# Attention, Fourier mixing and two feed-forward layers on one core: unrounded products gathered into three groups in the attention's loop

## The reference

```python
# batch 2, heads 8, sequence 768, head size 64
q_bits = (np.einsum('bhsd,dk->bhsk', q, proj) > 0)      # 6 bits each
k_bits = (np.einsum('bhsd,dk->bhsk', k, proj) > 0)
mask = q_bucket[:, :, :, None] == k_bucket[:, :, None, :]
scores = np.where(mask, scale * np.matmul(q, k.transpose(0, 1, 3, 2)), -1e9)
scores = scores - np.max(scores, axis=-1, keepdims=True)
attn = np.exp(scores)
attn = attn / (np.sum(attn, axis=-1, keepdims=True) + 1e-09)
out = np.matmul(attn, v)
# then: x = Fourier transform over tokens and features (real part), layer norm, 512 -> 2048 -> 512 feed-forward
# then: 512 -> 1024, gelu, gate mixed over the 768 tokens, 512 -> 512, residual
```

## Time and profile before

| what | value |
|---|---|
| median of 3 runs | 731.67 us (729.86 to 733.08) |
| profiled execution | 731.51 us, its span 729.7 us |
| TensorE, weight loads | 98%, 81% busy |
| VectorE, ScalarE, GpSimd | 66%, 52%, 48% busy |

### The profile page before, as it was taken

The page is one execution under the profiler, slowest core; times in us unless marked ns, Lnnn a source line. Parts: engine busy times, 40 slices in busy tenths (PEclk is TensorE's granted clock), DMA queues, the critical chain, the costliest instruction groups (busy, mean ns, idle before and its releaser), DMA issues.

```text
span 729.7 us, 11758 instructions
## 1 busy us (share of the span) xinstructions
PE 715.2 (98%) x3905; PEld 589.8 (81%) x3905; DVE 479.7 (66%) x701; ACT 382.3 (52%) x708; POOL 348.4 (48%) x341
## 2 busy tenths in 40 slices
PE   8999999999999999999999999999999998999998
PEld 8857666766676899988888888999998887888886
DVE  6877878778875799976555677444434774347533
ACT  4877887788785535554445445444541553025300
POOL 4178878887887910134533162536533353005500
PEclk9999999999999999999999999999999999999999
DMA  4332323332334140031211212721003000010001
GB/s 97 67 77 65 80 56 76 68 74 58 73 81 124 47 151 1 18 100 58 58 59 58 58 57 88 252 65 57 30 1 145 0 1 1 29 58 1 0 15 73
DMA packets 71076, 45.20 MB, mean 62 GB/s; under 512 B 44996, under 2 KB 61560, under 8 KB 70520
## 3 DMA queue, kind: packets, MB, share of 16 engines
q1 hardware_dynamic: 70456, 41.19, 20.7%
q0 software_dynamic: 576, 3.43, 1.4%
HBM read 35.42 MB, written 3.15 MB: 53 GB/s over the span
## 4 chain that ended last, share of the span: by engine, by line
PE 86%; DVE 8%; POOL 2%; ACT 2%; issue 1%; DMA 1%; SPq 0%; POOLq 0%; ACTq 0%; DVEq 0%
PE PS L811 81%; DVE un L2011 2%; DVE mneg L1773 1%; PE PS L835 1%; PE PS L1098 1%; PE PS L1315 1%; PE PS L1269 1%; DMA ops<-mrow 1%; PE PS L950 1%; PE PS L1260 1%; DVE st L1999 0%; DVE W1L L2044 0%; DVE ops L1744 0%; DVE ops L1765 0%; DVE ops L1738 0%
## 5 line engine op out<-in xcount | busy, mean ns | idle before, releaser
L811 PE MATMUL PS<-ops 98*128 98x384 f32 (+1 forms) x576 | 134.7, 359 | 3.4 <-DMA ops<-mrow 1.1
L811 PEld LDWEIGHTS PS<-ops 98*128 98x128 f32 (+1 forms) x576 | 95.2, 189 | 44.2 <-ACT E L1383 19.6
L1773 DVE TENSOR_REDUCE mneg<-PS 128x1 f32<-128x768 f32 x96 | 91.5, 956 | 36.8 <-PE PS L811 36.1
L1383 ACT ACTIVATE E<-PS 128x384 f32<-128x384 f32 x192 | 83.4, 486 | 44.6 <-PE PS L811 43.8
L661 POOL TENSOR_TENSOR esum<-esum,E 128x768 f32<-128x768 f32 x56 | 102.6, 1832 | 2.8 <-ACT E L1383 0.3
L646 POOL TENSOR_TENSOR W2L<-W2R,W2H 128x1024 fp32r<-128x1024 f32 x16 | 38.8, 2428 | 111.8 <-ACT W2H L1367 111.8
L2060 DVE SCALAR_TENSOR_TENSOR hL<-pre,hH 128x384 fp32r<-128x384 f32 x42 | 43.8, 1043 | 51.1 <-ACT hH L1628 51.1
L811 PE MATMUL PS<-BH,W1H 128*128 128x384 f32 x228 | 76.8, 337 | 0.4 <-DVE hL L2060 0.2
L811 PE MATMUL PS<-BH,W1L 128*128 128x384 f32 x228 | 76.8, 337 | 0.0
L811 PE MATMUL PS<-BL,W1H 128*128 128x384 f32 x228 | 76.1, 334 | 0.0
L811 PE MATMUL PS<-W2H,hH 128*128 128x512 f32 x192 | 75.5, 393 | 0.0
(11 more groups left out here) (211 smaller groups left out, 1595.4 us busy)
## 6 DMA issues: line engine op xcount, KB each, us to landing
W1R<-in_moe_w_ch_dram SPq DMA_DIRECT2D x32, 256.0 KB, 3.2
W2R<-in_moe_w_ch_dram SPq DMA_DIRECT2D x32, 256.0 KB, 3.0
ops<-ops SPq DMA_DIRECT2D x30, 192.0 KB, 3.0
qk<-in_k_dram SPq DMA_DIRECT2D x32, 96.0 KB, 2.5
qk<-in_q_dram SPq DMA_DIRECT2D x32, 96.0 KB, 2.6
vn<-in_v_dram SPq DMA_DIRECT2D x32, 96.0 KB, 2.5
out_dram<-X SPq DMA_DIRECT2D x12, 256.0 KB, 2.0
WsgR<-in_moe_w_sg_dram SPq DMA_DIRECT2D x1, 2304.0 KB, 8.0
```

Source lines behind the costliest of these rows:

```text
L811: return pe.matmul(dst, lhs, rhs, start=start, stop=stop, **kw)
L1383: act.activation(A["E"][:, e_slot(t, 0, kt), half(a)], PS[:, ST_BANK + a, 0:HALF], ACT.Exp, scale=EXP_SCALE).then_inc(exp_done, 1)
L1773: dve.tensor_reduce(A["mneg"][:, s, j:j + 1], PS[:, bank:bank + 2, 0:HALF], AX.XY, ALU.max, negate=True).then_inc(max_done, 1)
```

## The change

Two of the functions are changed, TensorE's and ScalarE's `one_time`, in the order of their steps alone. In TensorE's round the last max pair of head `t+1` goes ahead of the transposes, the denominators of head `t-1` go from behind the first max pair of head `t+2` to right behind the first part of the values, and the turn-back goes from the round's end to ahead of the second part of the values. In ScalarE's round the copy of the keys goes behind the third exponentials (tile 2), and the copy of the sums ahead of the fourth (tile 3) instead of behind them.

```diff
                 if t.has(0):
                     scores(t, 0, 2)
+                if t.has(1):
+                    scores_for_max(t, 1, 5)
                 if t.has(3):
                     transposes(t, 3)
-                if t.has(1):
-                    scores_for_max(t, 1, 5)
                 if t.has(0):
                     values(t, 0, 0)
+                if t.has(-1) and not late(t, -1):
+                    denominators(t, -1)
+                if t.has(0):
                     scores(t, 0, 3)
                 if t.has(2):
                     scores_for_max(t, 2, 0)
-                if t.has(-1) and not late(t, -1):
-                    denominators(t, -1)
                 if t.has(0):
                     scores(t, 0, 4)
...
                 if t.has(2):
                     scores_for_max(t, 2, 1)
+                if t.has(-1) and not late(t, -1):
+                    turn_back(t, -1)
                 if t.has(0):
                     values(t, 0, 1)
                     scores(t, 0, 5)
                 if t.has(2):
                     scores_for_max(t, 2, 2)
-                if t.has(-1) and not late(t, -1):
-                    turn_back(t, -1)
...
                 if t.has(2):
                     mask_rows(t, 2, 1)
-                if t.has(3):
-                    upper_keys(t, 3)
                 if t.has(0):
                     exponentials(t, 2)
                 if t.has(3):
+                    upper_keys(t, 3)
                     upper_queries(t, 3)
                 if t.has(1):
                     split_upper(t, 1)
+                if t.has(-1) and not late(t, -1):
+                    raw_sums(t, -1)
                 if t.has(0):
                     exponentials(t, 3)
-                if t.has(-1) and not late(t, -1):
-                    raw_sums(t, -1)
```

## The result

The changed kernel takes 737.73 us (median of 4, 737.32 to 739.26) against 730.76 for the kernel before on the same chip: ratio 1.0095, 95% interval 1.0078 to 1.0111. It is slower by 7.0 us; 739.2 was forecast, 7.5 above the median shown.

The account below looks back on a forecast made before the run. TensorE alone was taken to bound the attention loop. Terms -0.34 - 0.21 + 0.60 + 0.31 + 0.25 = +0.61 us a round, +7.3 in 12 rounds, +0.3 in the tail: 739.2 us forecast, range 735.0 to 743.0.

Parts of the forecast that it names:

- Bound: Attention loop, heads 1 to 12: each nanosecond TensorE saves or waits is a nanosecond of the kernel, twelve times over.
- Group price, -0.34: Denominators merged behind the values' first part on TensorE: one 64-wide group fewer saves its fixed price, 0.34 us a round.
- Rows' wait, -0.21: Scores behind the turn-back: with the sums' copy earlier, the wait for the rows' DMA goes, saving 0.21 us a round.
- Q+5.7: Next head's first scores: the maxima's rows arrive 5.7 us after scores 3 start; TensorE comes at 6.0, so no wait.
- Sixth maximum, +0.60: Sixth max pair on TensorE: waits for VectorE's reduction of the fifth, 0.50 plus 0.10 unhidden load, +0.60 us a round.
- Scores 4, +0.31: Scores 4 on TensorE: wait for exponentials 3 to free their bank, +0.31 us a round, bounds 0.14 and 0.40.
- Q+0.81: ScalarE: exponentials 3 start 0.81 us after scores 3 start, behind the sums' copy that now stands ahead of them.
- First scores and the next max pair, +0.25: Next head's scores 0 wait for exponentials 5, then max pair 3 for the maxima's cycle: +0.25 us a round, bounds 0.17, 0.30.
- Rival A: Attention loop: VectorE's and ScalarE's results are ready in time, only the two savings stand, -6.6 us, 725; chance 0.05.
- B: Rival, no change: only the sixth maximum is late, ScalarE hides the rest, 0.6 us more, 732; chance 0.10.
- C: Rival: merging the denominators saves nothing, their weights still cost a full group, 0.34 stays, 743.3 us; chance 0.05.
- VectorE cannot begin sooner: At the sixth max pair: VectorE's reduction of the fifth cannot start earlier, since VectorE already idles before it.

Follow-up runs that it names:

- e4: Against the kernel before, only the denominators moved behind the values' first part and the sums' copy ahead of exponentials 3: 728.14 us, ratio 0.9955.
- e9: Against e4, the sums' copy left behind exponentials 3 on ScalarE, as in the kernel before: 731.30 us, ratio 0.9995 to the kernel before.
- e1: Against the kernel before, only the sixth max pair moved ahead of the transposes: 738.25 us, ratio 1.0098.
- e2: Against the changed kernel, the sixth max pair put back behind the transposes: 731.96 us, ratio 1.0007 to the kernel before.
- e6: Against the kernel before, one unrounded product more a round, 64 wide with 64 columns, between scores 3 and the max pair: 737.36 us, ratio 1.0084.
- e7: Against the kernel before, one unrounded product more a round, 128 wide with 64 columns, between scores 3 and the max pair: 734.70 us, ratio 1.0048.

## Why the prediction was right

**Bound.** That a nanosecond of TensorE is one of the kernel held in every experiment: the rounds' differences times twelve give the differences at equal clock within 1 us (those of the medians within 1.5).

**Group price, -0.34.** Measured 1.44 + 0.80 + 0.08 + 0.10 - 2.08 = 0.34. The two other groups that the change dissolves had no price: the transposes none, the turn-back a wait.

**Rows' wait, -0.21.** Right in cause and size (e4), and e9 shows that it hangs on the place of ScalarE's copy, as the prediction said, and not on TensorE's order. The forecast place held too: in the changed kernel TensorE's queue has the rows at 101.71, 5.72 behind scores 3 (95.99), for the Q+5.7 forecast. That is 0.2 ahead of the exponentials that these scores then wait for (101.94); in e9 the rows have nothing to spare.

**Sixth maximum, +0.60.** Measured 0.62 alone (e1). It could be read off the last rounds of the trace before, where the same neighbours already stood.

**Scores 4, +0.31.** The mis-sized term, and half of its reason was wrong. Measured 2.12 - 1.85 = 0.27, and 0.24 by the starts of single instructions. The prediction let the sums' copy push exponentials 3 to Q+0.81. They start at Q+0.74 (95.99 to 96.73), and e9 shows them there without the copy as well: TensorE's own scores release them. With 0.74 the prediction's sum gives 0.24. That the denominators' cover is missing was right, that the copy adds to it was not.

```profile
96.11 0.69 ACT L1368 ACTIVATE sumT<-PS 128x384 f32<-128x384 f32 x1 [0.34 <-PE PS L811]
96.73 0.87 ACT L1384 ACTIVATE E<-PS 128x384 f32<-128x384 f32 x2
```

**First scores and the next max pair, +0.25.** Measured from scores 5 to the third max pair 103.18 - 100.78 = 2.40, for twelve products and 0.10, 2.20: 0.20, and 0.09 more inside the pair's record, which begins with its load.

**Sum.** +0.61 a round was forecast, +0.58 measured, +6.9 in twelve rounds for 7.3. The terms as measured add up to 0.54, or 0.63 with the 0.09; the trace tells no more than that. The last rounds cost 0.9 in the profile for the 0.3 forecast (the loop begins 0.4 earlier in the changed kernel's profile, so 7.5 + 0.4 - 6.9, rounded). Some of it stands at head 14, where scores 4 start 1.19 behind scores 3 (246.37 to 247.56) for 0.80 without a wait. For some the prediction had no term: in head 13's round no hash bits stand between the first and the second max pair, and the second starts 0.40 behind the rows' product (232.72 to 233.12, 0.18 idle for VectorE's maximum), where before it was 0.06. The rest is open. The two misses nearly cancel, and that is luck. The forecast time of 739.2 is 1.5 above the 737.73 for another reason: it starts from a kernel before with the slow stretch of the clock in it (731.5 and 731.7), and the changed kernel's executions mostly have none. The attention's +7.5 is the fair measure for the 7.6 of the sum. Rival A fell with e1, where one of the three waits alone costs more than the two savings. B needed the rest of the change to save 0.55 a round, and e2 saves 0.05. C fell with the 2.08.

**"VectorE cannot begin sooner"** was true, but half: in the changed kernel it also could not have begun much sooner by its own queue. An edit that starts the fifth pair earlier would find VectorE busy.

## What to carry to other kernels

Before gathering work of a kind, price each group by starts in the trace: here three groups were dissolved, one had a price, one had none, and one only seemed to have one, because a DMA came late behind it. Then ask what stood between two uses of a single buffer: work that is moved away from between them gives up cover, and a place in the trace where that cover is already missing (here the pipeline's last rounds) tells the price before the kernel is run. A copy in front of a DMA wants to be early in its engine's queue: moving it by one place was worth 0.26 a round (e4 against e9), nearly as much as the dissolved group. And before a microsecond of a median is explained, the granted clock of the executions in it has to be looked at: here it was worth up to 1.8 us, more than some of the edits.

## What the runs showed of the hardware

A lone unrounded product of 64 columns between rounded ones costs 0.45 us when its weights are 64 wide and 0.23 when they are 128 wide, though its place, its columns and the kind of its operands are the same. Six transposes in a row, 128 wide, cost 0.11 each and nothing on the way in or out. I had expected the short 128-wide one to be as free; what its further 0.1 is remains open, so a small price of the operands' kind is not excluded. The Trainium skill, "TensorEngine Tiling (Array Packing)", Key Properties, says that a change of the tiling mode drains the engine; the 0.22 between e6 and e7 and the 0.34 of a whole group agree with it.
